# Attention with top-k followed by a feed-forward layer: Mish and the split of its result by halves, two slots apart, and the down product two slots earlier

## The chip, the cores and the metric

The kernel runs on one core of a Trainium2 chip. The metric is the device time of one execution in microseconds (us); lower is better.

## The reference

Inputs are q, k and v of shape 4 x 8 x 576 x 64 (batch, heads, sequence, head size), `w_in` of 512 x 2048 and `w_out` of 2048 x 512, all float32. What is computed, cut to what matters:

```python
scores = q @ k.T / 8
kth = np.partition(scores, -32, axis=-1)[..., -32:-31]
scores = np.where(scores >= kth, scores, -1e9)
attn = exp(scores - max); attn = attn / (attn.sum() + 1e-9)
x = (attn @ v), heads side by side          # 2304 x 512
h = x @ w_in                                # 2304 x 2048
g = h * tanh(softplus(h))                   # Mish
y = g @ w_out                               # 2304 x 512
```

## The kernel before, in words

The 2304 rows of x are cut into 18 blocks of 128 rows. A block needs all 8 heads of its rows, taken in 4 "duos" of two tiles (a tile is 128 rows of one head against 576 keys), so that there are 72 duos. Each engine runs its own loop over slots s, one slot for each duo (`DUOS` is 72), and the offset of a step within the slots is written out by hand. Semaphores join the engines; every engine works through its own list strictly in the order written.

What happens to duo d, with the line numbers of the profile:

- PE computes the scores in slot d-2 (L314), three products each since q and k are split into a high and a low part. ACT copies them to `x_sb` in the same slot (L445).
- DVE finds the 32nd largest value of each row in its slot d, with eight-wide maxima and replacements (L558, L565, L573). POOL forms a limit and the negated maximum (`negate`, L615 and L617) in slot d+1, ACT forms a penalty (L456), POOL subtracts it (`exponents`, L624), ACT takes Exp (L464), POOL adds 1e-9 (`guard`, L628), all in slot d+1. DVE takes the reciprocal within its own slot d+2 (L548, some 3 us after the slot began), and POOL multiplies by it (`normalise`, L635).
- PE transposes in slot d+3 (L332), ACT copies to `pT` (L473), and PE multiplies by v for two duos together in the even slots (L350, L357). Blocks 4 and 13 are "mixed": they gather the last 64 rows of two batches; their scores are wider.
- After a block's fourth duo ACT copies x transposed to `xT` (L481).

The feed-forward part of block m is spread over slots as well. A group is a quarter of the 2048 hidden units:

- `up(m, j)`, PE, group j, 32 matmuls (L373): slot 6+4m+j. ACT copies it to `g_raw` one slot later (`copy_up`, L491).
- `mish(m)`, ACT, both halves of `g_raw` in place, one after the other (L498): slot 10+4m.
- `split_g(m, h)`, POOL, half h: a cast to `g_hi` (L608) and a subtraction to `g_lo` (L610): slots 11+4m and 12+4m.
- `down(m, j)`, PE, group j, 12 matmuls of 512 columns (L386): slot 12+4m+j. After the last group ACT copies `ps_y` to `y_sb` (`copy_y`, L504), and SP stores it (L258).

PE's order within a slot is: transposes, down, values (even slots), scores, up. The scores of slot s overwrite the PSUM that the transposes of the same slot wrote, so they wait until ACT has copied it (`pT_copied`). ACT's order is: copy_pT, penalties, split of q, copy_up, copy_xT, copy_x, copy_y, Exp, split of k, split of w_out, Mish. POOL's is: negate, split_g, split of w_out, normalise, exponents, split of q, guard, split of k. Splits of k for a new batch fall in slots 14 and 15, 30 to 33, and 50 and 51. PE's loop ends with slot 74. What is left of the feed-forward part stands behind the loops as a list: on PE down(15, 3), up(17, 1 to 3), the four groups of down(16), the four groups of down(17).

Of the kernel before, what the change touches and what calls it, by code (L numbers as in the profile page):

```python
# [8 lines left out]
ACT = mybir.ActivationFunctionType  # L9
# [6 lines left out]
PAIRS, PPB = B * H // 2, H // 2  # L16
# [4 lines left out]
FT, KC = FF // P, DM // P  # L21
GROUPS = 4
# [5 lines left out]
BLOCKS = B * S // P  # L28
DUOS = BLOCKS * PPB
# [7 lines left out]
LAG_EXP, LAG_NORM, LAG_PT = 1, 2, 3  # L37
# [1 line left out]
BLOW_UP = 2.0 ** 90  # L39
NEG = -3.0e38  # L40

UP_SLOT, MISH_SLOT, DOWN_SLOT = 6, 10, 12
WCHUNKS = 8
FPW = FT // WCHUNKS

# [36 lines left out]
def values_slot(s):  # L82

    return (s | 1) + LAG_PT
# [17 lines left out]


STAGED = PPB


def w_chunks_at(s):
# [7 lines left out]
def program(nc, k_in, q_in, v, w_in, w_out, y_out):  # L115
    with ExitStack() as ctx:
# [50 lines left out]
        wlo_ready = sem("wlo_ready")  # L167
# [52 lines left out]
        @block.sync  # L220
        def _(sp):
            def load_k(g):

                if g == PPB:
                    sp.wait_ge(klo0_ready, 1)
                elif g > PPB:
                    sp.wait_ge(klo_ready, 1 if g == PPB + 1 else g - RAWS)
                sp.dma_start(k_raw[:, g % RAWS, :], k_in[g, :, :]).then_inc(k_loaded[g % RAWS], 16)

            def load_q(s):  # L230
                if s > STAGED:
                    sp.wait_ge(qlo_ready, s)
                n = q_cols(s)
                sp.dma_start(q_raw[:, 0:n], q_in[s, :, 0:n]).then_inc(q_loaded, 16)

            def load_w(c):
                if c >= 2:
                    sp.wait_ge(wlo_ready, c - 1)
                rows = w_out[P * FPW * c:P * FPW * c + P * FPW, :].rearrange("(t p) n -> p t n", p=P)
                sp.dma_start(w_stage(c).rearrange("p (t n) -> p t n", t=FPW), rows).then_inc(wout_loaded[c % 2], 16)  # L240

            def load_v(pr, i):
                g, layout, _, _ = V_USES[pr][i]
                if i >= 1:

                    sp.wait_ge(out_ready, V_USES[pr][i - 1][3] + 1)
                sp.dma_start(v_sb[:, pr, :, :], v[g, layout, :, :].rearrange("p (k c) -> p k c", k=KV)
                             ).then_inc(v_loaded[pr], 16)

            def store(m):  # L250
                sp.wait_ge(y_copied, m + 1)
                if is_mixed(m):
                    for h in range(2):
                        t = S * (2 * (m // BPP) + h) + MIX_START
                        sp.dma_start(y_out[t:t + D, :], y_sb[D * h:D * h + D, :]).then_inc(y_stored, 16)
                else:
                    t = S * batch_of(m) + T_START[unit_of(m)]
                    sp.dma_start(y_out[t:t + P, :], y_sb[:, :]).then_inc(y_stored, 16)  # L258

            load_k(0)  # L260
            sp.dma_start(y_sb[:, :].rearrange("p (s c) -> p s c", s=STAGED),
                         q_in[0:STAGED, :, 0:P].rearrange("s p c -> p s c")).then_inc(q_staged, 16)
            load_k(1)
            for g in range(RAWS, PPB):
                sp.dma_start(k_source(g), k_in[g, :, :]).then_inc(k_staged[g - RAWS], 16)
            load_w(0)
            load_w(1)
            load_q(STAGED)
            for pr in range(PPB):
                load_v(pr, 0)  # L270
            load_k(PPB)
            load_k(PPB + 1)
            for k in range(KC):
                sp.dma_start(win[:, k, :], w_in[P * k:P * k + P, :]).then_inc(win_loaded, 16)
            for s in range(DUOS + DOWN_SLOT):
                if STAGED < s + 3 < DUOS:
                    load_q(s + 3)
                for c in w_chunks_at(s - 1):
                    if c + 2 < WCHUNKS:
                        load_w(c + 2)  # L280
                for g in splits_at(s - 1):
                    if PPB <= g and g + RAWS < PAIRS:
                        load_k(g + RAWS)
                for pr in range(PPB):
                    for i in range(1, len(V_USES[pr])):
                        if values_slot(V_USES[pr][i - 1][3]) == s:
                            load_v(pr, i)
                m, j = divmod(s - DOWN_SLOT, GROUPS)
                if j == GROUPS - 1 and 0 <= m < BLOCKS:
                    store(m)  # L290
            sp.wait_ge(y_stored, 16 * stores(BLOCKS - 1))

        @block.tensor
        def _(pe):
# [94 lines left out]
                mm.then_inc(down_ready, 1)  # L389

            pe.wait_ge(ident_ready, 1)
            for s in range(-2, DUOS + LAG_PT):
                if s >= LAG_PT:
                    transposes(s - LAG_PT)
                m, j = divmod(s - DOWN_SLOT, GROUPS)
                if m >= 0:
                    down(m, j)
                for d in (s - LAG_PT - 1, s - LAG_PT):
                    if d >= 0 and values_slot(d) == s:
                        values(d)  # L400
                if s + 2 < DUOS:
                    scores(s + 2)
                m, j = divmod(s - UP_SLOT, GROUPS)
                if m >= 0:
                    up(m, j)
            down(BLOCKS - 3, 3)
            for j in range(1, GROUPS):
                up(BLOCKS - 1, j)
            for j in range(GROUPS):
                down(BLOCKS - 2, j)  # L410
            for j in range(GROUPS):
                down(BLOCKS - 1, j)

        @block.scalar
        def _(act):
# [67 lines left out]
            def copy_up(m, j):  # L483
                n = GROUPS * m + j
                act.wait_ge(up_ready, n + 1)
                if n == 0:
                    act.wait_ge(wlo_ready, WCHUNKS)
                if j % 2 == 0 and m >= 1:

                    act.wait_ge(glo_ready, 2 * (m - 1) + j // 2 + 1)  # L490
                act.activation(g_raw[:, FPG * j:FPG * j + FPG, :], ps_u[:, n % 2, :, :],  # L491
                               ACT.Copy).then_inc(up_copied, 1)

            def mish(m):
                for h in range(2):
                    act.wait_ge(up_copied, GROUPS * m + 2 * h + 2)
                    g = g_raw[:, FT // 2 * h:FT // 2 * h + FT // 2, :]
                    act.activation(g, g, ACT.Mish).then_inc(mish_ready, 1)  # L498

            def copy_y(m):  # L500
                act.wait_ge(down_ready, GROUPS * m + GROUPS)
# [4 lines left out]
            split_k(0)  # L506
            split_q(0)
            split_k(1)
            for s in range(-2, DUOS + LAG_PT):
                if s >= LAG_PT:  # L510
                    copy_pT(s - LAG_PT)
                if 0 <= s - LAG_EXP < DUOS:
                    penalties(s - LAG_EXP)
                if s + 3 < DUOS:
                    split_q(s + 3)
                m, j = divmod(s - UP_SLOT - 1, GROUPS)
                if m >= 0:
                    copy_up(m, j)
                if s >= LAG_PT and (s - LAG_PT) % PPB == PPB - 1:
                    copy_xT((s - LAG_PT) // PPB)  # L520
                if 0 <= s + 2 < DUOS:
                    copy_x(s + 2)
                m, j = divmod(s - DOWN_SLOT, GROUPS)
                if m >= 0 and j == GROUPS - 1:
                    copy_y(m)
                if 0 <= s - LAG_EXP < DUOS:
                    exps(s - LAG_EXP)
                if s > -2:
                    for g in splits_at(s):
                        split_k(g)  # L530
                for c in w_chunks_at(s):
                    split_w(c)
                m, j = divmod(s - MISH_SLOT, GROUPS)
                if m >= 0 and j == 0:
                    mish(m)
            copy_up(BLOCKS - 1, 0)
            copy_y(BLOCKS - 3)
            for j in range(1, GROUPS):
                copy_up(BLOCKS - 1, j)
            mish(BLOCKS - 1)  # L540
            copy_y(BLOCKS - 2)
            copy_y(BLOCKS - 1)

        @block.vector
        def _(dve):
# [39 lines left out]
        def _(pool):  # L585
# [55 lines left out]
                               pattern=[[-1, P]], channel_multiplier=1).then_inc(ident_ready, 1)  # L641
            split_q(0)
            split_k(1)
            for s in range(-2, DUOS + LAG_NORM):
                if 0 <= s - LAG_EXP < DUOS:
                    negate(s - LAG_EXP)
                m, j = divmod(s - MISH_SLOT - 1, GROUPS)
                if m >= 0 and j < 2:
                    split_g(m, j)
                for c in w_chunks_at(s - 1):  # L650
                    split_w(c)
                if 0 <= s - LAG_NORM:
                    normalise(s - LAG_NORM)
                if 0 <= s - LAG_EXP < DUOS:
                    exponents(s - LAG_EXP)
# [4 lines left out]
                if s > -2:  # L660
                    for g in splits_at(s):
                        split_k(g)
            for m in range(BLOCKS - 2, BLOCKS):
                for h in range(2):
                    split_g(m, h)


# [37 lines left out]
```

## Time and profile before

| | |
|---|---|
| median of 3 runs | 783.95 us (783.53 to 784.21) |
| the profiled execution's own time | 782.78 us |
| its span, first to last instruction | 781.0 us |
| PE busy | 717.6 us (92%) |
| DVE busy | 700.3 us (90%) |
| ACT busy | 546.1 us (70%) |
| POOL busy | 546.3 us (70%) |
| mean granted clock of PE | 0.986 |

Times in the profile run from the start of the span. "PE" is the matmul part of TensorE and "PEld" its weight loads; a matmul's end is modelled, so PE's busy time says less than the distance from one start to the next. Bracketed text at the end of a row of the timeline is the engine's idle time before that row and what ended it.

### The profile page before, as it was taken

Reading aid. Unit: us, or ns where it says so; the run is one execution under the profiler, and the core shown is the slowest. Engines: PE = TensorE matmul, PEld = TensorE weight load, DVE = VectorE, ACT = ScalarE, POOL = GpSimd, SP = SyncE. Lnnn points to the kernel's source line nnn. Section 1 sums busy time; section 2 is a strip of 40 time slices with the busy share of each in tenths; the row PEclk is TensorE's granted clock in tenths of the full one; section 3 lists DMA queues with packets and bytes.
Section 4 is the critical chain, followed back from the end, with each engine's and each line's share of the span. In section 5 each row is a group of like instructions: output and inputs, shape, how many; then the busy total and the mean of one; then the engine's idle time right before and its main releaser. Section 6 shows DMA issues by size and latency. Waiting matters only on the chain.

```text
span 781.0 us, 16741 instructions
## 1 busy us (share of the span) xinstructions
PE 717.6 (92%) x6280; PEld 641.7 (82%) x6280; DVE 700.3 (90%) x1513; ACT 546.1 (70%) x994; POOL 546.3 (70%) x677
## 2 busy tenths in 40 slices
PE   2257759999999999999999999999999999999998
PEld 2246758988888888888888888988888888889896
DVE  6999999998999999999999999998999999996000
ACT  4677666776868687878686878686868686867420
POOL 3977568697767676887676768687767776767333
PEclk9987999999999999999999999999999999999999
DMA  9521000031121000211100000020122000000000
GB/s 346 185 62 34 8 8 12 15 115 40 59 85 45 8 22 10 52 38 54 42 23 8 23 8 21 16 77 23 56 75 90 8 22 8 21 2 14 2 14 28
DMA packets 22689, 34.64 MB, mean 44 GB/s; under 512 B 2384, under 2 KB 11600, under 8 KB 22096
## 3 DMA queue, kind: packets, MB, share of 16 engines
q1 hardware_dynamic: 22608, 33.56, 13.4%
q8 instruction: 50, 0.82, 0.4%
q14 instruction: 31, 0.25, 0.1%
HBM read 28.84 MB, written 4.72 MB: 43 GB/s over the span
## 4 chain that ended last, share of the span: by engine, by line
PE 55%; DVE 32%; POOL 4%; ACT 4%; issue 4%; DMA 1%; SPq 0%; ACTq 0%; POOLq 0%
PE ps_u L373 22%; PE ps_y L386 16%; DVE left L565 15%; DVE top L573 12%; PE ps_s L314 5%; PE ps_s L332 5%; PE ps_o L357 5%; DVE top L558 5%; POOL p_sb L624 1%; PE ps_o L350 1%; ACT p_sb L464 1%; POOL g_lo L610 1%; ACT pT L473 1%; POOL p_sb L635 1%; POOL k_lo L588 1%
## 5 line engine op out<-in xcount | busy, mean ns | idle before, releaser
L573 DVE MAX8 top<-left 128x8 f32<-128x576 f32 x432 | 305.2, 751 | 0.0
L373 PE MATMUL ps_u<-xT,win 128*128 128x128 f32 x2304 | 275.6, 278 | 2.6 <-ACT xT L481 2.6
L373 PEld LDWEIGHTS ps_u<-xT,win 128*128 128x128 f32 x2304 | 263.9, 192 | 13.0 <-issue 9.2
L565 DVE MATCH_REPLACE8 left<-top,left 128x576 f32<-128x576 f32 x288 | 212.5, 748 | 0.0
L624 POOL TENSOR_TENSOR p_sb<-x_sb,p_sb 128x576 f32<-128x576 f32 x144 | 200.8, 1416 | 0.0
L464 ACT ACTIVATE p_sb<-p_sb,neg_max 128x576 f32<-128x576 f32 x144 | 111.3, 775 | 62.0 <-POOL p_sb L624 61.5
L635 POOL TENSOR_SCALAR p_sb<-p_sb,recip 128x576 f32<-128x576 f32 x144 | 106.2, 748 | 51.0 <-DVE recip L548 51.0
L386 PE MATMUL ps_y<-w_hi,g_hi 128*128 128x512 f32 x288 | 119.0, 413 | 0.7 <-ACT y_sb L504 0.7
L445 ACT ACTIVATE x_sb<-ps_s 128x576 f32<-128x576 f32 x144 | 85.6, 648 | 48.0 <-PE ps_s L314 47.8
L386 PE MATMUL ps_y<-w_hi,g_lo 128*128 128x512 f32 x288 | 113.0, 392 | 0.0
L386 PE MATMUL ps_y<-w_lo,g_hi 128*128 128x512 f32 x288 | 112.3, 390 | 0.0
L456 ACT ACTIVATE p_sb<-x_sb,limit 128x576 f32<-128x576 f32 x144 | 103.5, 770 | 8.2 <-POOL limit L615 8.2
L565 DVE MATCH_REPLACE8 left<-top,x_sb 128x576 f32<-128x576 f32 x144 | 106.3, 749 | 0.0
L558 DVE MAX8 top<-x_sb 128x8 f32<-128x576 f32 x144 | 101.4, 748 | 3.0 <-ACT x_sb L445 3.0
L473 ACT ACTIVATE pT<-ps_s 128x512 f32<-128x512 f32 (+1 forms) x144 | 84.6, 638 | 23.3 <-PE ps_s L332 23.3
L332 PE MATMUL ps_s<-ident,p_sb 128*128 128x128 f32 x648 | 85.7, 279 | 8.8 <-POOL p_sb L635 7.6
L610 POOL TENSOR_TENSOR g_lo<-g_raw,g_hi 128x1024 fp32r<-128x1024 f32 x36 | 86.0, 2389 | 3.1
L357 PEld LDWEIGHTS ps_o<-pT,v_sb 128*64 128x64 f32 x1280 | 72.0, 141 | 18.1 <-issue 13.7
L357 PE MATMUL ps_o<-pT,v_sb 128*64 128x128 f32 x1280 | 80.9, 282 | 6.1 <-ACT pT L473 6.1
L332 PEld LDWEIGHTS ps_s<-ident,p_sb 128*128 128x128 f32 x648 | 75.2, 144 | 10.4 <-ACT x_sb L445 5.9
L314 PE MATMUL ps_s<-k_hi,q_hi 64*128 64x288 f32 (+1 forms) x288 | 43.1, 362 | 42.1 <-ACT pT L473 21.4
L314 PEld LDWEIGHTS ps_s<-k_hi,q_hi 64*128 64x128 f32 (+1 forms) x288 | 25.5, 199 | 60.4 <-issue 43.6
(41 smaller groups left out, 730.1 us busy)
## 6 DMA issues: line engine op xcount, KB each, us to landing
v_sb<-v_in SPq DMA_DIRECT2D x32, 320.0 KB, 3.6
g_raw<-w_out SPq DMA_DIRECT2D x8, 512.0 KB, 3.8
win<-w_in SPq DMA_DIRECT2D x4, 1024.0 KB, 11.8
y_out<-y_sb SPq DMA_DIRECT2D x16, 256.0 KB, 2.0
k_raw<-k_in SPq DMA_DIRECT2D x14, 288.0 KB, 2.9
q_raw<-q_in SPq DMA_DIRECT2D x60, 64.0 KB, 1.8
q_raw<-q_in SPq DMA_DIRECT2D x8, 128.0 KB, 2.1
p_sb<-k_in SPq DMA_DIRECT2D x2, 288.0 KB, 5.2
```

The lines of the kernel that those rows point to most:

```text
L314: mm = pe.matmul(ps_s[:, t, h, 0:HALF], q[r, s % QS, c:c + P], k[r, g % PPB, HALF * h:HALF * h + HALF], start=first, stop=final, skip_grou ...
L332: mm = pe.transpose(flat[:, P * k:P * k + P], p[:, P * k:P * k + P], ident[:, :])
L357: mm = pe.matmul(ps_o[D * h:D * h + D, j, :], v_sb[:, j, k, D * h:D * h + D], pT[:, s % 2, SPLIT_AT * h + k, :], start=(k == 0), stop=(k = ...
L373: mm = pe.matmul(ps_u[:, n % 2, i, :], win[:, k, P * f:P * f + P], xT[:, k, :], start=(k == 0), stop=(k == KC - 1), skip_group_check=True)
L386: mm = pe.matmul(ps_y[:, :], g[:, f, :], w[:, f, :], start=(f == 0 and g is g_hi and w is w_hi), stop=(f == FT - 1 and g is g_lo), skip_gr ...
L456: act.activation(p_sb[:, s % PS_, t, :], x_sb[:, s % XS, t, :], ACT.Relu, bias=limit[:, s % TS, t:t + 1], scale=-BLOW_UP).then_inc(penalty ...
L464: act.activation(p, p, ACT.Exp, bias=neg_max[:, s % TS, t:t + 1], scale=SCALE, accum_out=denom[:, s % TS, t:t + 1]).then_inc(exp_ready, 1)
L558: dve.max(best[:, t, 0:EIGHT], x[t]).then_inc(top8_ready, 1)
L565: dve.match_replace(out=left[:, t, :], in_to_replace=best[:, t, EIGHT * r:EIGHT * r + EIGHT], in_values=x[t] if r == 0 else left[:, t, :], ...
L573: dve.max(best[:, t, EIGHT * r + EIGHT:EIGHT * r + 2 * EIGHT], left[:, t, :]).then_inc(found, 1)
L624: pool.tensor_tensor(p, x_sb[:, s % XS, t, :], p, ALU.subtract).then_inc(arg_ready, 1)
L635: pool.tensor_scalar(p, p, recip[:, s % TS, t:t + 1], 1.0, ALU.mult, ALU.mult).then_inc(p_ready, 1)
```

## The change

The Mish of a block is taken by halves in two slots, 8+4m and 10+4m; each half is split one slot after its Mish, in slots 9+4m and 11+4m; the down product takes slots 10+4m to 13+4m. All loops but SP's own preamble and DVE's run to slot 81 (`SLOTS` is 82), and the lists behind the loops are gone, so that PE does one up and one down group in each of slots 75 to 77 and down groups alone in 78 to 81. `copy_y` and the store of a block follow its last down group, two slots earlier than they did. ACT's first `copy_up` waits for seven of the eight pieces of `w_lo` and its third for all eight, where the first waited for all eight.

```diff
-UP_SLOT, MISH_SLOT, DOWN_SLOT = 6, 10, 12
+UP_SLOT, MISH_SLOT, DOWN_SLOT = 6, 8, 10
+SLOTS = DOWN_SLOT + DUOS
...
+def group_at(s, first):
+    m, j = divmod(s - first, GROUPS)
+    return (m, j) if 0 <= m < BLOCKS else (None, None)
+
+def half_at(s, first):
+    m, j = group_at(s, first)
+    return (m, j // 2) if m is not None and j % 2 == 0 else (None, None)
...
 # SP
-            for s in range(DUOS + DOWN_SLOT):
+            for s in range(SLOTS):
...
 # PE
-            for s in range(-2, DUOS + LAG_PT):
-                if s >= LAG_PT:
+            for s in range(-2, SLOTS):
+                if LAG_PT <= s < DUOS + LAG_PT:
                     transposes(s - LAG_PT)
-                m, j = divmod(s - DOWN_SLOT, GROUPS)
-                if m >= 0:
+                m, j = group_at(s, DOWN_SLOT)
+                if m is not None:
                     down(m, j)
...
-            down(BLOCKS - 3, 3)
-            for j in range(1, GROUPS):
-                up(BLOCKS - 1, j)
-            for j in range(GROUPS):
-                down(BLOCKS - 2, j)
-            for j in range(GROUPS):
-                down(BLOCKS - 1, j)
...
 # ACT
-                if n == 0:
-                    act.wait_ge(wlo_ready, WCHUNKS)
+                if m == 0 and j % 2 == 0:
+                    act.wait_ge(wlo_ready, WCHUNKS - 1 + j // 2)
...
-            def mish(m):
-                for h in range(2):
-                    act.wait_ge(up_copied, GROUPS * m + 2 * h + 2)
-                    g = g_raw[:, FT // 2 * h:FT // 2 * h + FT // 2, :]
-                    act.activation(g, g, ACT.Mish).then_inc(mish_ready, 1)
+            def mish(m, h):
+                act.wait_ge(up_copied, GROUPS * m + 2 * h + 2)
+                g = g_raw[:, FT // 2 * h:FT // 2 * h + FT // 2, :]
+                act.activation(g, g, ACT.Mish).then_inc(mish_ready, 1)
...
-                m, j = divmod(s - MISH_SLOT, GROUPS)
-                if m >= 0 and j == 0:
-                    mish(m)
-            copy_up(BLOCKS - 1, 0)
-            copy_y(BLOCKS - 3)
-            for j in range(1, GROUPS):
-                copy_up(BLOCKS - 1, j)
-            mish(BLOCKS - 1)
-            copy_y(BLOCKS - 2)
-            copy_y(BLOCKS - 1)
+                m, h = half_at(s, MISH_SLOT)
+                if m is not None:
+                    mish(m, h)
...
 # POOL
-                m, j = divmod(s - MISH_SLOT - 1, GROUPS)
-                if m >= 0 and j < 2:
-                    split_g(m, j)
+                m, h = half_at(s, MISH_SLOT + 1)
+                if m is not None:
+                    split_g(m, h)
...
-            for m in range(BLOCKS - 2, BLOCKS):
-                for h in range(2):
-                    split_g(m, h)
```

## Rows read from the trace of the kernel before

**Rows 1.** Busy by windows: PE, PEld, DVE, ACT, POOL, then clock, DMA share, GB/s.
```profile
602.98:641.70 38.72, 38.72 (x342) 34.54 (x344) 38.72 (x85) 29.40 (x55) 28.00 (x37) 1.00 0.04 15
```

**Rows 2.** Chain of waits in order of time: start, us, what; behind slot 74.
```profile
744.46 10.72 PE ps_u L373 x96
755.17 10.91 PE ps_y L386 x48
766.75 11.19 PE ps_y L386 x48
```

**Rows 3.** Timeline of ACT and POOL at the end: start, us, instruction.
```profile
755.70 2.00 ACT L498 ACTIVATE g_raw<-g_raw 128x1024 f32<-128x1024 f32 x2
...
760.77 1.04 POOL L608 CAST g_hi<-g_raw 128x1024 fp32r<-128x1024 f32 x1 [12.71 <-PE ps_y L386]
761.88 2.39 POOL L610 TENSOR_TENSOR g_lo<-g_raw,g_hi 128x1024 fp32r<-128x1024 f32 x1
```

**Rows 4.** Timeline of PE, slots 9 to 11 where it stood idle, and slot 12.
```profile
94.90 0.53 PE L314 MATMUL ps_s<-k_hi,q_hi 64*128 64x288 f32 x4 [2.71 <-ACT pT L473]
...
104.52 1.31 PE L357 MATMUL ps_o<-pT,v_sb 128*64 128x128 f32 x20 [2.22 <-ACT pT L473]
...
108.04 3.84 PE L373 MATMUL ps_u<-xT,win 128*128 128x128 f32 x32 [1.21 <-ACT xT L481]
...
117.62 0.70 PE L314 MATMUL ps_s<-k_hi,q_hi 64*128 64x288 f32 x4 [4.76 <-ACT pT L473]
...
123.83 1.15 PE L332 MATMUL ps_s<-ident,p_sb 128*128 128x128 f32 x9
```

**Rows 5.** Busy by windows as in rows 1, inside slot 11.
```profile
118.00:120.00 2.00, 2.00 (x15) 1.72 (x12) 2.00 (x6) 1.89 (x5) 2.00 (x3) 0.50 0.00 0
```

**Rows 6.** Timeline of POOL, the normalise of slot 11.
```profile
119.00 1.47 POOL L635 TENSOR_SCALAR p_sb<-p_sb,recip 128x576 f32<-128x576 f32 x2
```

**Rows 7.** Timeline of ACT around a Mish of block 8, and in the slot behind it.
```profile
430.16 1.28 ACT L498 ACT_TABLE_LOAD   x1
431.45 2.02 ACT L498 ACTIVATE g_raw<-g_raw 128x1024 f32<-128x1024 f32 x2
433.37 1.18 ACT L473 ACTIVATE pT<-ps_s 128x512 f32<-128x512 f32 x2
...
439.03 1.28 ACT L464 ACT_TABLE_LOAD   x1 [0.64 <-POOL p_sb L624]
...
446.81 1.19 ACT L445 ACTIVATE x_sb<-ps_s 128x576 f32<-128x576 f32 x2 [1.77 <-PE ps_s L314]
```

**Rows 8.** The same stretch on PE, POOL and DVE.
```profile
434.87 0.53 PE L314 MATMUL ps_s<-k_hi,q_hi 64*128 64x288 f32 x4
...
442.04 0.22 POOL L628 TENSOR_SCALAR denom<-denom 128x2 f32<-128x2 f32 x1 [1.30 <-ACT p_sb L464]
...
443.38 0.17 DVE L548 RECIPROCAL recip<-denom 128x2 f32<-128x2 f32 x1
```

**Rows 9.** Groups of ACT by form: count, busy us, mean ns, idle before.
```profile
L498 ACT ACT_TABLE_LOAD x17 | 21.8, 1283 | 0.3
L464 ACT ACT_TABLE_LOAD x16 | 20.5, 1283 | 11.9 <-POOL p_sb L624 11.9
```

**Rows 10.** Waits at the three changes of batch: windows 100:185, 300:345, 500:540.
```profile
DVE recip L548 <- POOL denom L628: 4.4, 2, 2.9
...
DVE recip L548 <- POOL denom L628: 1.1, 1, 1.1
PE ps_s L314 <- ACT pT L473: 1.2, 2, 0.9
...
DVE recip L548 <- POOL denom L628: 3.7, 2, 2.8
PE ps_s L314 <- ACT pT L473: 1.8, 2, 1.0
```

**Rows 11.** Timeline of PE at the first change of batch, slot 15.
```profile
159.50 0.77 PE L314 MATMUL ps_s<-k_hi,q_hi 128*128 128x288 f32 x4 [0.96 <-ACT pT L473]
```

More of the change, by code:

```diff
@@ L287, in _ @@
                             load_v(pr, i)
-                m, j = divmod(s - DOWN_SLOT, GROUPS)
-                if j == GROUPS - 1 and 0 <= m < BLOCKS:
+                m, j = group_at(s, DOWN_SLOT)
+                if m is not None and j == GROUPS - 1:
                     store(m)
@@ L391, in _ @@
             pe.wait_ge(ident_ready, 1)
-            for s in range(-2, DUOS + LAG_PT):
-                if s >= LAG_PT:
+            for s in range(-2, SLOTS):
+                if LAG_PT <= s < DUOS + LAG_PT:
                     transposes(s - LAG_PT)
-                m, j = divmod(s - DOWN_SLOT, GROUPS)
-                if m >= 0:
+                m, j = group_at(s, DOWN_SLOT)
+                if m is not None:
                     down(m, j)
                 for d in (s - LAG_PT - 1, s - LAG_PT):
-                    if d >= 0 and values_slot(d) == s:
+                    if 0 <= d < DUOS and values_slot(d) == s:
                         values(d)
@@ L402, in _ @@
                     scores(s + 2)
-                m, j = divmod(s - UP_SLOT, GROUPS)
-                if m >= 0:
+                m, j = group_at(s, UP_SLOT)
+                if m is not None:
                     up(m, j)
-            down(BLOCKS - 3, 3)
-            for j in range(1, GROUPS):
-                up(BLOCKS - 1, j)
-            for j in range(GROUPS):
-                down(BLOCKS - 2, j)
-            for j in range(GROUPS):
-                down(BLOCKS - 1, j)
         @block.scalar
@@ L508, in _ @@
             split_k(1)
-            for s in range(-2, DUOS + LAG_PT):
-                if s >= LAG_PT:
+            for s in range(-2, SLOTS):
+                if LAG_PT <= s < DUOS + LAG_PT:
                     copy_pT(s - LAG_PT)
@@ L515, in _ @@
                     split_q(s + 3)
-                m, j = divmod(s - UP_SLOT - 1, GROUPS)
-                if m >= 0:
+                m, j = group_at(s, UP_SLOT + 1)
+                if m is not None:
                     copy_up(m, j)
-                if s >= LAG_PT and (s - LAG_PT) % PPB == PPB - 1:
+                if LAG_PT <= s < DUOS + LAG_PT and (s - LAG_PT) % PPB == PPB - 1:
                     copy_xT((s - LAG_PT) // PPB)
@@ L522, in _ @@
                     copy_x(s + 2)
-                m, j = divmod(s - DOWN_SLOT, GROUPS)
-                if m >= 0 and j == GROUPS - 1:
+                m, j = group_at(s, DOWN_SLOT)
+                if m is not None and j == GROUPS - 1:
                     copy_y(m)
@@ L532, in _ @@
                     split_w(c)
-                m, j = divmod(s - MISH_SLOT, GROUPS)
-                if m >= 0 and j == 0:
-                    mish(m)
-            copy_up(BLOCKS - 1, 0)
-            copy_y(BLOCKS - 3)
-            for j in range(1, GROUPS):
-                copy_up(BLOCKS - 1, j)
-            mish(BLOCKS - 1)
-            copy_y(BLOCKS - 2)
-            copy_y(BLOCKS - 1)
+                m, h = half_at(s, MISH_SLOT)
+                if m is not None:
+                    mish(m, h)
         @block.vector
@@ L643, in _ @@
             split_k(1)
-            for s in range(-2, DUOS + LAG_NORM):
+            for s in range(-2, SLOTS):
                 if 0 <= s - LAG_EXP < DUOS:
                     negate(s - LAG_EXP)
-                m, j = divmod(s - MISH_SLOT - 1, GROUPS)
-                if m >= 0 and j < 2:
-                    split_g(m, j)
+                m, h = half_at(s, MISH_SLOT + 1)
+                if m is not None:
+                    split_g(m, h)
                 for c in w_chunks_at(s - 1):
                     split_w(c)
-                if 0 <= s - LAG_NORM:
+                if 0 <= s - LAG_NORM < DUOS:
                     normalise(s - LAG_NORM)
```

## The prediction

> **What bounds the kernel now.** I read the busy shares first: PE and DVE at 92% and 90% of the span, ACT and POOL at 70%. Then the windows: over exactly four slots in the middle PE and DVE are both busy for the whole 38.72 us, 9.68 us a slot, while ACT has 29.40 and POOL 28.00 [rows 1]. So two engines bound the body together. The reader should look for an idle gap on either; in steady slots there is none, and a step moved within them costs PE nothing, because it is the same work elsewhere.
>
> The chain of waits shows what follows. Behind slot 74 it is PE alone: three up groups in 10.72 us, four down groups in 10.91, a gap from 766.08 to 766.75 in which down(17) waits for the copy of down(16)'s result, and four more in 11.19 [rows 2]. PE reaches this list only when DVE has long ended, so each down group that stands there costs its full time.
>
> The third view is PE's timeline before down starts, slots 9 to 11. PE is idle there for 2.71, 2.22, 1.21 and 4.76 us, 10.9 in all [rows 4]. The fourth is the waits at the three places where keys of a new batch are split: DVE stands 4.4, 1.1 and 3.7 us, 9.2 in all, for a reciprocal's input, and PE 1.2 and 1.8 at the last two for ACT's copy of pT [rows 10].
>
> **The end.** The change lets PE do down groups in slots 10 and 11, so each later down group moves up two slots. After up(17, 0) PE has three ups and seven downs, where it had three ups and nine. One down is 10.91/4 = 2.73 us [rows 2], two are 5.46. The 0.67 us gap goes too: down(16, 3) now stands ahead of up(17, 3), a group of 3.57 us, and ACT's copy fits under it.
>
> A new dependency takes the gap's place: the last half of g needs up(17, 3). Before, down(16) hid that. From the end of the up to the start of Mish was 0.53 us (755.17 to 755.70), one half of Mish is 1.0, cast and subtraction run from 760.77 to 764.27, 3.5 us [rows 2, 3]. With 0.1 to 0.2 for handing over it is 5.2 us, and the first two groups of down(17) take 5.46: hidden, with 0.3 to spare. No table is loaded there, as no Exp stands between the last Mishes. If that cover failed, an overrun would show one for one. **Term: -6.1** (bounds -6.4 and -5.1, the latter if the handovers cost 1 us more).
>
> **The start.** The two downs go to slots 10 and 11. Of the idle time there 2.22 + 1.21 + 4.76 = 8.2 us lies in those slots [rows 4], against 5.46 of work. But it is not all free. Mish of half 0 now comes in slot 8 and pushes ACT's copy of pT in slot 9 by a table load and a half, 1.28 + 1.0 = 2.3 us [rows 7]; PE waits for just that copy in slot 9, so its slot 10 begins 2.3 late. In slot 10 the down group fills the 2.22 and most of the rest; in slot 11 Mish is one half, not two, so that the copy comes 1.0 earlier than at 117.6. I follow the steps: slot 10's transposes at 102.2, its up at 110.0, slot 11's transposes 113.8, its down until 117.7, scores, then up. Before, PE had been idle 4.76 us and its granted clock was 0.50 (the lower level, 1.2 GHz) in the window behind it [rows 5]; scores and up took 6.2 us together (117.62 to 123.83), where an up at the upper level took 3.84 [rows 4] and the scores some 1.1 by PE's slot of 9.68. With PE busy I expect the upper level, and slot 12 at 122.7 in place of 123.83. **Term: -1.1.** Bounds: the data of slot 12's transposes were ready at 120.47 [rows 6], so no more than -3.4; if only the later wait and not the earlier ones took work, 5.46 + 2.3 less 4.76 = +3.0.
>
> **Steady slots.** Mish and Exp need different tables. Loads were 17 and 16 [rows 9]. Halves in slots 8, 10, ... 72 each load Mish's, and the Exp behind all but the last loads its own back: 33 and 32, so 32 more loads of 1.283 us, 41 us more on ACT, which goes from 70% to some 76%. What hides them: in the Mish slot, load and both halves ended at 433.4, the copy of pT at 434.55, and PE's scores began at 434.87, 0.3 us of margin [rows 7, 8]. A slot with one half has 1.0 more. In the slot behind, split, Exp's load, Exp and guard put the sum ready at 442.26 for a reciprocal at 443.38, a margin of 1.1 [rows 8]. That pattern came once in four slots and now comes in each two. It closes: two slots later ACT stood 1.77 us idle for PE's scores [rows 7], and POOL no longer has its second split of 3.5 us in that slot, so the two extra loads start from the same phase each time. **Term: 0**, priced further among the rivals.
>
> Here the Trainium skill speaks against the change. In the trace a load takes 1.28 us and Mish begins 0.01 behind it (430.16, 431.45) [rows 7]. ScalarE: Activation LUTs, section What ACT_TABLE_LOAD costs, gives every switch of set about 2.66 us, a load and a drain of 1.38. By that figure, an estimate, the 32 switches would be 85 us of ACT and the total some 22 us longer where half of the drains reach the path. The trace shows no such gap, and I take its 1.28.
>
> **Changes of batch.** In slots 14 to 16 POOL had two splits of k in each of two slots and a half of g in each of 15 and 16. Now the halves are in 13, 15 and 17: the relief of slot 16 is 3.5 us, more than the 2.9 that DVE lost there [rows 10]. ACT's Mish in slot 14 is half, so PE's wait for pT there should go; it was 0.96 us at 159.50, one of two [rows 11]. But slot 17 now has a split and a load, 3.5 + 1.28 = 4.8 us, where it had neither; less the relief of 3.5 that leaves 1.3 late. Slots 50 to 53 are the same. In 30 to 33 there is one split of k a slot, and two Exp loads fall among them where one did: I take half a load, 0.6, as lost. PE's waits were 1.2 and 1.8 at the last two [rows 10], and I take twice the 0.96 for the first: 4.9 in all. I take 1.3 - 1.9 = -0.6, then +0.6, then 1.3 - 1.8 = -0.5. **Term: -0.5**; bounds -4.9 (all gone) and +4.9 (all doubled). A gain of DVE alone ends nothing, since PE's chain ends last.
>
> **Queues.** SP's wait for a block's y, with the store, moves from slot 15+4m to 13+4m; behind it stand the loads of q for the next slot, and then of k and v. The wait lasts until the down group of the same slot, as before, and those were in time behind the same wait; cost 0. POOL's waits: each split waits up to 1 us for its half of Mish, twice a block in place of once, within POOL's 30% idle; who waits behind it is normalise, whose result was 3.4 us early for PE (120.47 against 123.83) [rows 4, 6]. Slot 73 is alike: a split now stands ahead of the last normalise, and if it is late next, the last transposes are. ACT's wait for the last piece of w_lo becomes shorter; 0. DVE has no edit.
>
> **Sum.** -6.1 - 1.1 - 0.5 = -7.7. Span 781.0 - 7.7 = 773.3; the profiled execution's 782.78 becomes 775.1; it stood 1.17 below the median, so I predict a median of 776.2.
>
> **Rivals.**
> - **All waits go.** POOL's relief removes PE's waits at the batch changes as well and the start gives its full 3.4: -6.1 - 3.4 - 4.9 = -14.4, 769.6. For it: the relief is larger than the stalls. Against: three more loads in each of those stretches. Anywhere from 769.6 to 773.5: 0.17.
> - **The end alone.** Table loads at the start and at batch changes give back what the relief brings, +0 to +4: 778.5 to 782. For it: the margin of 1.1. 0.20.
> - **Slower: the Exp loads on DVE's path.** Place: the 16 new slots in which Exp's load stands between POOL's subtraction and the reciprocal. If the margin of 1.1 isn't rebuilt within two slots, each costs up to its 1.28, 20.5 in all: 783.95 - 6.1 + 20.5 = 798. It decides from 0.4 us each (16 x 0.4 = 6.4, more than the end brings). Against: ACT's 1.77 us of idle time. The page's switch cost would lead here, and its chance is in this one: 0.07.
> - **The shift is empty.** PE is late by all of it in slots 10 and 11, so the two downs are only paid earlier: +3.0 at the start, and some loss at the batch changes: -6.1 + 3.0 + 2 to 4, about 783 to 785. 0.06.
> - **My forecast**, 773.5 to 778.5: 0.50.
>
> About 0.2% (1.6 us) is what a measurement of this kernel can tell from no change. Faster by more takes in the forecast, all waits go and the end alone: 0.87; within 0.06; slower 0.07. The range from 770.5 to 781.5 holds the forecast and most of its two neighbours, 0.8.
>
> **What would show it.** Right: behind up(17, 0) the chain shows up and down in turn and four downs at the end, with no gap before down(17, 0) or down(17, 2). Slot 12 begins near 122.7 at full clock. Table loads 33 and 32, each 1.28. DVE's wait for guard falls below 9.2 before the end. PE's scores wait for pT no more in steady slots. Wrong: waits of DVE for guard or of PE for pT at every second slot (the slower rival), a gap of microseconds behind the table loads, or slot 12 later than 124.

## The result, and the profile after

The changed kernel takes 774.46 us (median of 4 runs, 774.0 to 775.45) against 783.74 for the kernel before in the same comparison: a ratio of 0.9884, 95% interval 0.9868 to 0.9900, or 9.3 us. The forecast was 776.2, in a range of 770.5 to 781.5. The profiled execution took 774.75 us with a span of 773.0, where before it was 782.78 and 781.0.

The busy times of the changed kernel, from the first part of its page:

```profile
PE 718.6 (93%) x6280; PEld 642.3 (83%) x6280; DVE 700.3 (91%) x1513; ACT 583.5 (75%) x1026; POOL 547.0 (71%) x677
```

Only ACT has more to do, 37 us. The same window as in [rows 1], PE, PEld, DVE, ACT, POOL:

```profile
602.98:641.70 38.72, 38.72 (x346) 34.54 (x342) 38.72 (x85) 31.72 (x56) 27.92 (x37) 1.00 0.05 15
```

PE and DVE are as full as they were, and ACT has 31.7 us instead of 29.4. The extra work fits into ACT's idle time.

ACT's groups by form, which answer to [rows 9]:

```profile
L506 ACT ACT_TABLE_LOAD x33 | 42.3, 1283 | 0.6
L472 ACT ACT_TABLE_LOAD x32 | 41.1, 1283 | 57.6 <-POOL p_sb L625 57.6
```

33 and 32 loads of 1.283 us, as counted ahead. The end of the chain of waits, which answers to [rows 2] (start, us, what):

```profile
748.89 3.57 PE ps_u L388 x32
752.46 2.73 PE ps_y L401 x12
755.20 3.57 PE ps_u L388 x32
758.77 11.14 PE ps_y L401 x48
```

Ups and downs alternate, from 735.98 on, four downs close the list, and nothing stands idle between the pieces. PE ends at 769.91; before it was 777.94.

To see where the time went I read from the timelines when PE began the transposes of each slot. These are the differences to the kernel before, in us; the two profiles of the changed kernel differ in this by 0.14 at most. The last two columns belong to runs described below.

| PE reaches | before, at | changed | halves only | before, no loads |
|---|---|---|---|---|
| slot 10 | 99.88 | +4.54 | +0.19 | +1.39 |
| slot 12 | 123.83 | -0.05 | -0.71 | -0.03 |
| slot 18 | 186.27 | -1.12 | -1.80 | -0.71 |
| slot 30 | 302.69 | -1.12 | -1.80 | -0.70 |
| slot 37 | 372.94 | -0.77 | -1.47 | -1.77 |
| slot 50 | 497.61 | -0.77 | -1.46 | -1.77 |
| slot 56 | 560.07 | -1.87 | -2.50 | -2.45 |
| slot 74 | 730.91 | -1.87 | -2.51 | -2.45 |
| end of the last down | 777.94 | -8.03 | -2.48 | -2.44 |

The column of the changed kernel reads: nothing at the start, -1.1 at the first change of batch, +0.3 at the second, -1.1 at the third, exactly nothing in all slots between them, and -6.2 behind slot 74.

### The profile page after: what moved, and what is told of

Same layout as the page of the kernel before. It is cut to its first block, busy times and chain, and to the rows that moved or that the text cites. A ratio compares the mean times of both kernels' runs of the same rounds, so it can differ in the third digit from the quotient of the medians.

```text
span 773.0 us, 16774 instructions
## 1 busy us (share of the span) xinstructions
PE 718.6 (93%) x6280; PEld 642.3 (83%) x6280; DVE 700.3 (91%) x1513; ACT 583.5 (75%) x1026; POOL 547.0 (71%) x677
## 4 chain that ended last, share of the span: by engine, by line
PE 55%; DVE 35%; POOL 4%; issue 3%; ACT 3%; DMA 0%; SPq 0%; ACTq 0%
PE ps_u L388 22%; DVE left L566 17%; PE ps_y L401 16%; DVE top L574 13%; PE ps_s L329 5%; PE ps_s L347 5%; DVE top L559 5%; PE ps_o L372 5%; PE ps_o L365 1%; POOL g_lo L611 1%; POOL p_sb L625 1%; POOL p_sb L636 1%; ACT p_sb L472 1%; ACT L472 0%; ACT k_hi L432 0%
## 5 line engine op out<-in xcount | busy, mean ns | idle before, releaser
L629 POOL TENSOR_SCALAR denom<-denom 128x2 f32<-128x2 f32 x72 | 15.9, 221 | 100.4 <-ACT p_sb L472 100.4
L609 POOL CAST g_hi<-g_raw 128x1024 fp32r<-128x1024 f32 x36 | 37.4, 1040 | 67.7 <-ACT g_raw L506 67.7
L472 ACT ACT_TABLE_LOAD x32 | 41.1, 1283 | 57.6 <-POOL p_sb L625 57.6
```

Source lines behind the costliest of these rows:

```text
L472: act.activation(p, p, ACT.Exp, bias=neg_max[:, s % TS, t:t + 1], scale=SCALE, accum_out=denom[:, s % TS, t:t + 1]).then_inc(exp_ready, 1)
```

## The experiments

Theory: the down groups that moved from the end into PE's idle time at the start are most of the gain; the halves relieve POOL and ACT at the changes of batch; table loads are hidden in steady slots. Rivals: the halves are the gain; or the loads cost much and the shift hides it. The variants ran on three chips, and each ratio is to the kernel before on the same chip. The changed kernel took 774.46 us in the first comparison and 774.26 when it was run again beside the second group; differences "to the changed kernel" are to one of these two, 0.2 us apart.

**The changed kernel again.**

> The changed kernel unedited, on the same chip as the variants beside it: 774 to 775.5.

774.26 us (4 runs, 773.86 to 775.28). Its profile puts PE at most 0.14 us from the first one at every slot, but its four executions spread over 1.4 us. So differences of medians below about 1 us say little by themselves, and a position of PE in a trace says more.

**Halves only.**

> The changed kernel with the slots set back: Mish of a half in slots 10+4m and 12+4m, its split one slot later, down in slots 12+4m to 15+4m as before. So Mish and split by halves two slots apart and the 32 more table loads are kept, and the down product does not move. My theory (the down product's two slots are the gain at the end, 5.5 of 6.2 us): behind up(17, 0) PE takes three ups and nine downs, 35.1 us; the end is shorter than the kernel before by the 0.7 us gap alone, and with 1 to 2 us from the changes of batch the whole is 1 to 3 us faster than the kernel before, 781 to 783. Slot 12 of PE stays near 123.8. Rival (the halves are the gain, by evening out ACT and POOL): 775 to 778. Rival (the table loads cost on the path and the shift hides it): slower than before, 785 to 790.

```diff
-UP_SLOT, MISH_SLOT, DOWN_SLOT = 6, 8, 10
+UP_SLOT, MISH_SLOT, DOWN_SLOT = 6, 10, 12
```

The edit also puts ACT's wait for `w_lo` in the first `copy_up` back to all eight pieces. That wait does not show: PE begins slots 8 and 9 within 0.1 us of where the changed kernel does.

780.34 us, ratio to the kernel before 0.9957 (0.9944 to 0.9971). That is 0.7 us below the 781 to 783 of my theory, and both rivals fell: with 31 and 32 table loads, nearly all of the new ones, the kernel is still 3.4 us faster by the ratio, and it is 5.9 slower than the changed kernel. The column above parts it: -0.7 at the start, -1.8 in all at the batch changes, and from slot 74 on nothing. The end of its chain:

```profile
758.13 5.47 PE ps_y L401 x24
...
764.28 11.19 PE ps_y L401 x48
```

I had expected the 0.7 us gap to go. It is still there, from 763.60 to 764.28: with down in slots 12 to 15 nothing stands between down(16, 3) and down(17, 0), interleaved or not. So the gap belongs to the shift as well. From slot 74 to the end PE needs 47.03 us in the kernel before, 47.06 here and 40.87 in the changed kernel. Against halves only, the shift of the down product is worth 6.2 us there and costs 0.7 at the start.

**No table loads, before and after.**

> The kernel before with Relu in place of Mish (the output then holds relu instead of Mish in g). Relu is served by the table that Exp uses, so the 33 table loads go and nothing else changes. If table loads are hidden in slots beside PE and DVE, the time stays within 2 us of before, what goes being the part at the changes of batch: 780 to 783.5. If each load lay on the path by its 1.28 us it would be 742.

> The changed kernel with Relu in place of Mish (the output then holds relu instead of Mish in g): 65 table loads fewer. My theory: steady slots hide them, so 1 to 4 us less than the changed kernel (770 to 773.5), all of it in slot 9 (PE's idle time of 5.1 us there shrinks to under 4) and at the changes of batch. Rival (the loads eat into the gain at every second slot): more than 6 us less, under 768.

```diff
-act.activation(g, g, ACT.Mish)
+act.activation(g, g, ACT.Relu)
```

Both kernels leave out Mish, and g holds Relu. 779.93 us (0.9944 of the kernel before, 0.9930 to 0.9958) and 769.45 (0.9813, 0.9800 to 0.9826). Both lie just below the ranges that I gave (780 to 783.5 and 770 to 773.5), far from the rivals. In both traces a single table load is left, the one at the program's start. So 33 loads cost 4.4 us by the medians (784.30 in that comparison) and 2.4 by the end of PE's work in the profiles, 65 loads 5.0 and 5.3, out of 42 and 83 us of ACT's time. They cost where the trace has no slack: before, -0.7, -1.1 and -0.7 at the three changes of batch and at most 0.03 in the slots between; in the changed kernel, against itself, -2.2 at slots 10 to 12, then -0.4, -1.7 and -1.0 at the batch changes, 5.3 in all, and again at most 0.03 between. The steady slots do hide them.

**Mish by quarters.**

> The changed kernel with Mish taken by quarters, one in each slot 7+4m to 10+4m, the splits and the down product where they are. Table loads go from 65 to about 131, one of each kind in every slot, 85 us more on ACT. It looks for the point at which loads come onto the path. In a slot ACT then has some 7 us of its other work, 0.6 of Mish and 2.6 of loads, 10.2 us against PE's and DVE's 9.7: I expect ACT to be the bound and 10 to 40 us more than the changed kernel, 785 to 815. If ACT's overlap of instructions and its idle time still cover it, within 2 us of the changed kernel, 774 to 777.

```diff
-                m, h = half_at(s, MISH_SLOT)
+                m, j = group_at(s, UP_SLOT + 1)
                 if m is not None:
-                    mish(m, h)
+                    mish(m, j)
```

831.32 us, 57 more than the changed kernel, and more than I gave it. The trace has 66 and 65 loads. PE falls back in every stretch, by about 0.75 us a slot between the batch changes. DVE's wait for guard, from the list of waits of the whole execution (total, times, longest):

```profile
DVE recip L549 <- POOL denom L629: 65.9, 37, 8.0
```

ACT is busy in only 81% of the span, yet from 487.52 to 502 its timeline has no gap above 0.02 us: the loads stand in a chain with work that DVE waits for. The rival "slower" has its price here: it is what happens when both loads fall in each slot.

**Early Exp.** The reload of Exp's table begins only when ACT's wait for POOL has ended. The changed kernel has 57.6 us of idle time before those 32 loads, in the row of the groups above. A small Exp ahead of the wait draws the load forward.

> The changed kernel with an Exp of one column into a scratch tile ahead of the real Exp, in each odd slot behind a Mish. Exp's table load stands behind ACT's wait for POOL in the trace of the changed kernel (57.6 us of idle time before 32 loads, 1.8 us each); the small Exp lets the load run inside that idle time. My theory (the loads cost only at the changes of batch, where they come between POOL's subtraction and the guard): 1 to 2.5 us less, 772 to 773.5, DVE's waits for guard at the changes of batch shorter, slot 12 unchanged since the load in slot 8 is Mish's. Rival (it is ACT's busy time and not the place of the load that counts): 0 to 1 us more, 774 to 775.5.

```diff
+        early = sb("early", [P, 2])
...
+                if s > MISH_SLOT and s % 2 and s - LAG_EXP < DUOS:
+                    act.activation(early[:, s // 2 % 2:s // 2 % 2 + 1],
+                                   limit[:, (s - LAG_EXP) % TS, 0:1], ACT.Exp, scale=0.0)
                 if 0 <= s - LAG_EXP < DUOS:
                     exps(s - LAG_EXP)
```

771.43 us (0.9847 of the kernel before, 0.9834 to 0.9860), 3 us less than the changed kernel, somewhat better than expected. Its timeline of ACT in slot 43, the slot behind the Mish of [rows 7]:

```profile
433.73 1.28 ACT L536 ACT_TABLE_LOAD   x1
435.02 0.20 ACT L536 ACTIVATE early<-limit 128x1 f32<-128x1 f32 x1
435.60 0.78 ACT L473 ACTIVATE p_sb<-p_sb,neg_max 128x576 f32<-128x576 f32 x1 [0.37 <-POOL p_sb L628]
```

The load runs at once and the real Exp waits for POOL alone. There are as many loads and ACT is busy for 592.4 us in place of 583.5, and yet the kernel takes less time: here the place of a load counts, and not ACT's busy time. PE is 0.7, 1.4 and 0.7 us earlier than in the changed kernel at the three changes of batch; the 0.5 at the start go with the clock, since the up of slot 9 took 4.80 in place of 5.44 behind the same idle time.

> Mish by quarters, with the early Exp in every slot. By quarters took 831.3, 57 us more than the changed kernel, though ACT was busy only 81% of the span; so not its busy time but the chain through load, Exp, guard and reciprocal should set the slot. If so, taking Exp's load out of that chain gives back at least half: 780 to 805. If ACT's time is what bounds it, under 5 us change: 826 to 833.

806.73 us. Of the 57 us by which quarters are slower 25 come back, less than the half I expected, and PE still falls behind by some 0.4 us a slot. The chain is a good part of it and not all. ACT is busy in 85% of the span here; whether the rest is ACT's time alone stays open.

**The start.**

> The changed kernel with the very first half of Mish, block 0's in slot 8, put behind ACT's copy of pT in slot 9. My theory of the start: that Mish with its table load delays the copy of pT by 2.3 us, PE idles 5.1 us in one piece, its granted clock falls and the next up takes 5.4 us, and that is why slot 12 of PE did not come earlier than before. Then here PE's idle time in slot 9 is 2.7 us, the up takes 3.8, and slot 12 begins at 120.5 to 122 in place of 123.8; the time falls by 1 to 3 us where PE bounds the body, 771.5 to 773.5. Rival (DVE and POOL hold PE back by the first change of batch): slot 12 earlier, slot 18 not, and the time within 0.5 us of the changed kernel.

```diff
                     copy_pT(s - LAG_PT)
+                if s == MISH_SLOT + 1:
+                    mish(0, 0)
...
-                if m is not None:
+                if m is not None and s > MISH_SLOT:
                     mish(m, h)
```

First the changed kernel, PE in slot 9 and at the start of slot 10, which answers to [rows 4], and its clock, which answers to [rows 5]:

```profile
97.41 0.85 PE L329 MATMUL ps_s<-k_hi,q_hi 64*128 64x288 f32 x4 [5.11 <-ACT pT L481]
...
99.15 5.44 PE L388 MATMUL ps_u<-xT,win 128*128 128x128 f32 x32
104.42 1.15 PE L347 MATMUL ps_s<-ident,p_sb 128*128 128x128 f32 x9
```

```profile
98.00:100.00 2.00, 2.00 (x15) 1.72 (x13) 2.00 (x6) 2.00 (x5) 2.00 (x2) 0.50 0.00 0
```

The down groups filled the idle time of slots 10 and 11, but Mish in slot 8 made one piece of 5.1 us in slot 9, and behind it the clock was at its lower level. The slow up moved from slot 11 to slot 9. With the first Mish late:

```profile
95.10 0.53 PE L329 MATMUL ps_s<-k_hi,q_hi 64*128 64x288 f32 x4 [2.73 <-ACT pT L481]
...
102.48 1.17 PE L347 MATMUL ps_s<-ident,p_sb 128*128 128x128 f32 x9 [2.55 <-POOL p_sb L638]
```

The idle time is 2.73 and the up behind it took 3.84, at full clock. But a new wait of 2.55 us comes in slot 10: the split of g, now later, stands ahead of normalise on POOL. Slot 12 begins at 122.51, 1.3 us earlier where I had expected 1.8 to 3.3, and those 1.2 to 1.3 us stay to the end at each slot. The rival (held up at the first change of batch) falls by that. The time is 773.51 us against 774.26, at the weak end of what I expected.

This run doesn't price the clock. In the combined version without early Exp, below, the same up took 4.88 us behind 2.72 us of idle time, at the lower level, and slot 10 began at 102.48 all the same, since there too it waits for normalise. Nor does the length of the idle piece alone settle the clock: behind pieces of 2.71 to 2.75 us in slot 9 four profiles show the up at 3.84 us and three at 4.54 to 4.88. Behind 5.09 to 5.11 us, in all five profiles that have such a piece, it took 4.80 to 6.04.

These five (the changed kernel twice, early Exp, splits of k in even slots, down behind up) do price it. From the start of slot 9 to that of slot 12 they take 31.97, 32.48, 32.60, 32.63 and 33.19 us, with that up at 4.80, 5.30, 5.42, 5.44 and 6.04: what the up loses arrives in slot 12 in full. At 3.84 us, by the same line, slot 12 of the changed kernel would begin at some 122.2 (an estimate).

**Splits of k in even slots.**

> The changed kernel with the splits of k for new batches moved out of the slots in which POOL splits g: k pairs 6 and 7 in slot 16 instead of 15, 8 to 11 in slots 30, 32, 34, 36 instead of 30 to 33, 14 and 15 in slot 52 instead of 51. DVE's wait for guard at the three changes of batch was 1.3, 0.6 and 1.8 us after the change (without counting the ends of the loops) and should fall below 1.5 in all. My theory (PE bounds the body and ends the chain): the time moves by less than 1 us, 773.5 to 775. Rival (DVE's stalls at the batch changes carry to the end): 2 to 3.5 us less, 771 to 772.5.

```diff
+SPLIT_SLOT.update({6: 16, 7: 16, 8: 30, 9: 32, 10: 34, 11: 36, 14: 52, 15: 52})
```

772.00 us against 774.26. My theory said under 1 us and is wrong; PE gains 0.7, 1.7 and 0.7 us at the three places, 3.1 in the profile, which fell on the fastest execution of this version. The rival's size was right and its cause was not: DVE still waits 1.3 and 1.9 us at the first and third. The changed kernel shows it in slot 34, on POOL, ACT and PE:

```profile
344.72 1.41 POOL L589 TENSOR_TENSOR k_lo<-k_raw,k_hi 128x576 fp32r<-128x576 f32 x1 [0.34 <-ACT k_hi L432]
346.48 1.45 ACT L464 ACTIVATE p_sb<-x_sb,limit 128x576 f32<-128x576 f32 x2 [0.77 <-POOL limit L616]
348.51 0.58 ACT L489 ACTIVATE xT<-ps_o 128x512 f32<-128x512 f32 x1
349.14 3.84 PE L388 MATMUL ps_u<-xT,win 128*128 128x128 f32 x32 [1.06 <-ACT xT L489]
```

A split of k keeps POOL from the limit, ACT waits for that with the copy of x transposed queued behind it, and PE stands 1.06 us for the copy. With the splits in slots 32 and 34 and none in 33, ACT is early for the copy, at 345.70, and waits 0.22 us for PE itself; the up follows at 346.57 without a wait. Without table loads the same stretch lost nothing either, with the split of k left in slot 33. So it takes both, the load and the split of k in one odd slot, to make PE wait there.

**Together.**

> Both edits. If PE's start is held back later by POOL and DVE at the changes of batch, the two together give more than their sum: 770 to 772. If they are independent, the sum of the two. If PE's work alone bounds the rest, the same as the late first Mish alone.

770.46 us, ratio to the kernel before 0.9839 (0.9825 to 0.9854). PE is 4.3 us ahead of the changed kernel at slot 74, about the sum of 1.2 and 3.2: in the traces the two are independent. By the medians both together give 3.8 us and the two alone 0.8 and 2.3, but that surplus is within the spread of the executions.

> The two edits that helped (first Mish behind the copy of pT, splits of k in even slots) with the early Exp. The version without early Exp took 770.5. If moving the splits of k has already taken the stalls that the loads made, the early Exp adds nothing: 770 to 771. If some are left: 769 to 770.

769.92 us, ratio 0.9825 (0.9812 to 0.9839). It is the fastest version that computes the reference, 13.6 us below the kernel before and 4.5 below the changed one. The early Exp alone gave 3 us and gives 0.5 here, with intervals that overlap. The traces place those 0.5: PE is 0.75 earlier at slot 12, where the early load brings the copy of pT in slot 10 forward, and gains nothing more at the three changes of batch. There it and the moved splits remove the same lateness.

**Down behind up.**

> The changed kernel with one pair swapped at the end: in slot 77 PE takes up(17, 3) before down(16, 3). The copy of y of block 16 then has no cover, and the gap of 0.7 us before down(17, 0) should return, 0.4 to 0.9 us more, 774.7 to 775.4; the 0.3 us in which PE's weight load waited for g_lo should go. Rival (the wait for g_lo is the larger of the two): less than the changed kernel.

```diff
-                if m is not None:
+                if m is not None and s != DUOS + 5:
                     down(m, j)
...
                     up(m, j)
+                if s == DUOS + 5:
+                    down(BLOCKS - 2, GROUPS - 1)
```

775.26 us. The chain at the end:

```profile
749.40 7.14 PE ps_u L388 x64
756.55 2.75 PE ps_y L401 x12
...
759.97 11.19 PE ps_y L401 x48
```

The gap is back, 759.30 to 759.97, and from slot 74 to the end PE needs 41.61 us instead of 40.87: +0.74, as expected. By the medians the whole is 0.8 to 1.0 us more. In the profile PE ends 1.2 us later, of which 0.5 arose in slot 9 already, with the clock; the chain shows the swap's part. The weight load's wait of 0.3 us for g_lo went with it, so in the changed kernel the cover of the last split is just about used up.

## Why the prediction was right

- **The end.** -6.1 was forecast, 47.03 less 40.87 is 6.16. Down behind up shows the gap's part, 0.7; halves only shows that all 6.2 belong to the shift, which leaves 5.5 for the two down groups. The cover for the last half of g had 0.3 us to spare by the forecast; the trace has 0.3 us of waiting by a weight load and no gap between matmuls.
- **The start.** -1.1 was forecast, -0.05 came. The step that failed is "PE waits for just that copy in slot 9, so its slot 10 begins 2.3 late": the delay was priced as delay only. I had looked for the lower clock in slot 11 alone, and there it was at the upper level, as I had written. But 2.3 us of delay and the 2.7 us of idle time that stood in slot 9 made one piece of 5.11, and behind it the clock was at 0.50. Scores and up in slot 9, with what follows them until slot 10, took 7.01 us (97.41 to 104.42) where they had taken 4.98 (94.90 to 99.88). So slot 10 began at 104.42 where I had 102.2. Slots 10 and 11 won half of that back, and slot 12 began at 123.78. The two downs were paid out of idle time, and the 1.1 us that I expected on top was lost with the clock, as the five profiles above bear out.
- **Steady slots.** 0 was forecast. Between slots 18 and 30, 37 and 50, and 56 and 74 PE's difference does not change by more than 0.01, with 41 us more of loads. The kernels without loads show the same for all 65.
- **Changes of batch.** -0.6, +0.6 and -0.5 were forecast, -1.1, +0.3 and -1.1 came. DVE's wait for guard in the three windows of [rows 10]:

```profile
DVE recip L549 <- POOL denom L629: 1.3, 1, 1.3
...
DVE recip L549 <- POOL denom L629: 0.6, 1, 0.6
...
DVE recip L549 <- POOL denom L629: 1.8, 1, 1.8
```

  3.7 us in place of 9.2. Halves only has the same differences at all three places, so they come from the halves and not from the shift. The traces show two parts of it at the first. In slot 15 ACT's copy of pT comes at 157.21 in place of 158.18, since the Mish ahead of it is one half, and PE's wait of 0.96 is gone. In slot 17 it comes at 178.59 in place of 179.74, since POOL reached the normalise of slot 16 at 171.17 in place of 174.68 and so ACT the Exp that stands ahead of the copy, and PE's wait of 0.82 is gone. Both reliefs were forecast.

  The term was mis-sized: against them I had set 1.3 us as lost in slot 17, and again in 53, and what came onto PE's path was a new wait of 0.45 us in slot 16 and of 0.49 in 52. At the second change the wait of 1.06 us for the copy of x transposed, above, made the loss. "A gain of DVE alone ends nothing" was true but misleading, since POOL's lateness holds PE too, by way of ACT: moving the splits of k gave 2.3 us by the medians and 3.1 in the profiles.
- **The table load.** The Trainium skill (ScalarE: Activation LUTs, What ACT_TABLE_LOAD costs) would have made each switch about 2.66 us. In all profiles here the loads of Mish and Exp take 1.283 us each, with the next activation 0.01 us behind. No such drain lies ahead of them either: with the early Exp each of the 65 begins within 0.03 us of the end of the instruction before it. The measurement decides, and the trace's figure was the right one to take.
- **Sum.** -7.7 was forecast for the span, -8.0 came. Two errors of opposite sign, 1.1 us too good at the start and 1.3 too cautious at the batch changes, nearly cancelled. That is luck: the total is closer than its parts. The end, which is most of it, and the steady slots were right in size and in cause.

## What to carry to other kernels

In a software pipeline whose steady slots are full, look at both ends: here two down groups, moved forward from PE's tail into PE's idle time at the start, gave their full duration at the end and cost 0.7 us at the start. Extra work on an engine with idle time need not cost anything: 41 us of loads cost nothing in the steady slots. What cost was its place, ahead of something that the bounding engines wait for. Before moving a step into an idle stretch, see whether it joins two waits into one, and look at the engine's granted clock behind the joined wait.

## What was not expected of the hardware

A table load stands behind the semaphore wait of the activation that needs it: 32 loads with 57.6 us of idle time right before them, the loads themselves 41 us. With a one-column Exp of 0.20 us ahead, the 32 loads waited 0.6 us in all, and the kernel was 3 us faster. And a chain through ACT held up the kernel by much of 57 us with ACT busy in only 81% of the span, as Mish by quarters showed.

PE's clock behind an idle piece was not the same each time: behind 2.7 us in slot 9 it fell in three profiles and stayed up in four. The same source code ran with that up at 5.44 us in one execution and at 5.30 in another.
